# Moving seven output-tile additions in VectorE's order at the start of an MLP

## The reference

```python
def _moe_ref(x, w_in, w_out, a, b):     # x 1152 x 512, w_in 512 x 2048, w_out 2048 x 512
    h = x @ w_in
    h2 = h * h
    h3 = h2 * h
    P = a[0] + a[1] * h + a[2] * h2 + a[3] * h3
    Q = 1.0 + np.abs(b[0]) * np.abs(h) + np.abs(b[1]) * h2
    g = P / (Q + 1e-06)
    return g @ w_out
```

## Time and profile before

| | us |
|---|---|
| median of three runs | 685.32 |
| lowest, highest | 683.48, 688.41 |
| the profiled execution | 685.32 |
| its span (first to last instruction) | 683.5 |
| TensorE busy | 671.2 |
| VectorE busy | 513.4 |
| ScalarE busy | 410.5 |
| GpSimd busy | 443.7 |

### The profile page before, as it was taken

How to read it: one execution, slowest core, us unless ns; L and a number is a source line. 1 busy time by engine, 2 the same in 40 slices (tenths; PEclk the granted TensorE clock), 3 DMA queues, 4 the chain that set the end, 5 groups by cost and what they waited for, 6 DMA issues and landing times.

```text
span 683.5 us, 11834 instructions
## 1 busy us (share of the span) xinstructions
PE 671.2 (98%) x3940; PEld 623.7 (91%) x3940; DVE 513.4 (75%) x1005; ACT 410.5 (60%) x860; POOL 443.7 (65%) x440
## 2 busy tenths in 40 slices
PE   7899999999999999999999999999999999999998
PEld 5899999999999999988999999899999999999996
DVE  6899999999999958989899889977544444444432
ACT  5787887888887878998888888844511111111110
POOL 5877998999999979999789789845614440000000
PEclk9999999999999999999999999999999999999999
DMA  8567467666645430110110110122111100000012
GB/s 230 186 163 205 131 173 220 192 185 156 200 145 159 105 88 3 62 31 32 62 62 0 63 62 5 58 99 87 61 63 62 62 0 1 1 0 1 1 61 78
DMA packets 26012, 60.76 MB, mean 89 GB/s; under 512 B 3304, under 2 KB 7920, under 8 KB 25840
## 3 DMA queue, kind: packets, MB, share of 16 engines
q1 hardware_dynamic: 25680, 59.87, 29.6%
q10 hardware_dynamic: 288, 0.33, 0.2%
HBM read 43.78 MB, written 2.40 MB: 68 GB/s over the span
## 4 chain that ended last, share of the span: by engine, by line
PE 90%; DVE 3%; ACT 2%; DMA 2%; issue 1%; POOL 1%; SPq 0%; DVEq 0%; POOLq 0%; ACTq 0%
PE hb L909 31%; PE ob L966 24%; PE sc L811 11%; PE sc L819 9%; PE misc L837 5%; PE pv_ps L837 5%; PE tb L909 4%; DVE neg_part L1208 1%; DMA km_lo<-kqB 1%; DMA qrawA<-in_q 1%; DVE pt_lo L1217 0%; PE tb L903 0%; ACT num L1104 0%; ACT squares L1132 0%; DMA o_part<-o_sb 0%
## 5 line engine op out<-in xcount | busy, mean ns | idle before, releaser
L1039 ACT ACTIVATE pt_hi<-sc 128x384 fp32r<-128x384 f32 x216 | 90.4, 492 | 46.6 <-PE sc L819 46.6
L1208 DVE TENSOR_REDUCE neg_part<-sc 128x1 f32<-128x384 f32 x216 | 107.7, 549 | 11.5 <-PE sc L811 10.3
L1217 DVE TENSOR_TENSOR pt_lo<-sc,pt_hi 128x384 fp32r<-128x384 f32 x216 | 106.5, 548 | 2.4 <-ACT pt_hi L1039 1.4
L966 PE MATMUL ob<-wo_hi,gt_hi 128*128 128x512 f32 x252 | 99.6, 395 | 0.9 <-issue 0.9
L966 PE MATMUL ob<-wo_lo,gt_hi 128*128 128x512 f32 x252 | 99.2, 394 | 0.0
L966 PE MATMUL ob<-wo_hi,gt_lo 128*128 128x512 f32 x252 | 99.0, 393 | 0.0
L909 PE MATMUL hb<-xt_hi,wi_hi 128*128 128x384 f32 x280 | 94.6, 338 | 0.6 <-DVE xt_lo L1249 0.4
L909 PE MATMUL hb<-xt_lo,wi_hi 128*128 128x384 f32 x280 | 94.1, 336 | 0.0
L909 PE MATMUL hb<-xt_hi,wi_lo 128*128 128x384 f32 x280 | 94.0, 336 | 0.0
L1030 ACT ACTIVATE prob<-sc,neg_max 128x1152 f32<-128x1152 f32 x72 | 89.2, 1238 | 3.2 <-DVE neg_max L1210 3.2
L819 PE MATMUL sc<-ident,prob 128*128 128x128 f32 x648 | 83.1, 273 | 0.6 <-ACT prob L1030 0.6
(11 more groups left out here) (172 smaller groups left out, 1704.0 us busy)
## 6 DMA issues: line engine op xcount, KB each, us to landing
wraw<-in_moe_w_out SPq DMA_DIRECT2D x6, 1024.0 KB, 5.0
krawB<-in_k SPq DMA_DIRECT2D x8, 576.0 KB, 4.4
qrawB<-in_q SPq DMA_DIRECT2D x8, 512.0 KB, 5.7
krawA<-in_k SPq DMA_DIRECT2D x7, 576.0 KB, 4.4
o_part<-o_sb SPq DMA_DIRECT2D x14, 288.0 KB, 4.1
qrawA<-in_q SPq DMA_DIRECT2D x7, 512.0 KB, 5.9
wraw<-in_moe_w_in SPq DMA_DIRECT2D x3, 1024.0 KB, 5.2
wraw<-in_moe_w_gate SPq DMA_DIRECT2D x3, 1024.0 KB, 5.0
```

Source lines behind the costliest of these rows:

```text
L966: ins = nc.tensor.matmul(ob[(m + 1) % 2][:], gt[i][:, f, P * t:P * t + P], wo[c % 2][j][:, f, :], start=f == 0 and n == 0, stop=f == CHUNK ...
L1039: nc.scalar.activation(pt[0][:, 3 * c:3 * c + 3, PT_COL[i]:PT_COL[i] + P], src, ACT.Copy).then_inc(pt_hi, 1)
L1208: nc.vector.tensor_reduce(neg_part[:, s, c:c + 1], sc[s][:, c, 0:KBANK], AX.X, ALU.max, negate=True).then_inc(part_done, 1)
L1217: nc.vector.tensor_tensor(pt[1][:, kt, col], src, pt[0][:, kt, col].bitcast(F32), ALU.subtract).then_inc(pt_lo, 1)
```

## The change

The table of VectorE's turns goes, and `added(u)` is worked out from `behind`: up to u = 8 it takes what stands behind unit u + 1, at u = 9 nothing, and from u = 10 on what stands behind unit u.

```diff
-ADDED_AT = {5: 0, 6: 1, 7: 2, 10: 3, 11: 4, 13: 5, 14: 6}
...
         def added(u):
 
-            if u < 4 * CHUNK:
-                return [(0, ADDED_AT[u])] if u in ADDED_AT else []
-            return behind(u, 0)
+            return behind(u + 1, 0) if u <= 2 * CHUNK else behind(u, 0) if u > 2 * CHUNK + 1 else []
```

## The result

Before 685.18 us (median of 10 runs, 683.48 to 688.41), after 689.20 us (10 runs, 687.85 to 690.89). The ratio is 1.0054, with a 95% interval of 1.0037 to 1.0072: slower by 0.54%, 3.7 us (the medians differ by 4.0). The profiled execution took 688.53 us, 3.2 more than the profiled one of before, with a span of 686.7 against 683.5. The forecast was 687.8, in a range of 684.6 to 690.6.

The account below looks back on a forecast made before the run. TensorE's instruction stream was taken to bound the kernel. Terms +1.64 (tile 2), -0.22 (tile 3's old wait), +2.17 (tile 5) and -1.09 (old wait at 313.26) made +2.5 us on 685.32: 687.8, range 684.6 to 690.6.

Parts of the forecast that it names:

- Two waits: TensorE waits for VectorE's copies about 1.4 us before tile 2 and about 1.9 us before tile 5.
- The old gap at 313 us: TensorE's 0.88 us wait for lo(15) before chunk 1's tile 0 vanishes with its 0.21 restart: -1.09 us.
- GpSimd holds turn 6: activation1(5) waits for GpSimd's second product, so tile 0's copy ends at 276.02 and tile 2 is 1.64 us late.
- ScalarE holds turn 12: activation1(11) follows ScalarE's exponential of unit 11, ended at 294.29, so losing earlier copies makes turn 12 no earlier.
- the first stall: TensorE's stall before tile 2, +1.64 us, drops out of the total because tile 3's copy alone sets tile 5's end.
- the copy of tile 3: At the end of VectorE's turn 12, done at 297.0, it makes tile 5 end 3.59 us late; the largest term.
- The extra copy in turn 8: VectorE's added copy starts turn 9 some 0.6 us later and may push ScalarE by 0.1 to 0.2 us.
- upper bound, 3.7: Likeliest case from above: extra copies of turns 8 and 15 each push the chain by their full 0.6 us.
- The clock: TensorE's clock falls from 2.4 to 1.2 GHz after the stall at 295 us, giving 693 us; chance 0.04.
- near something that cost no clock: Waits of about 1.4 and 1.9 us resemble TensorE's 1.82 us standstill at 18.4 to 20.2 us, clock 1.00.
- Rival 1: VectorE's chain is less tied to ScalarE and GpSimd, both additions arrive in time; 684.0 us at best; chance 0.14.
- Rival 3: Lateness passes from TensorE through ScalarE to VectorE, so tiles 6 to 8 wait some 0.7 us each; 690; chance 0.07.

Follow-up runs that it names:

- the early half alone: Copies of tiles 0 to 2 in turns 6, 7, 8, those of tiles 3 to 6 left as in the kernel before; 684.69 us, ratio 1.0014 to the kernel before.
- the second profile of the changed kernel: Profiled execution of the changed kernel measured again, with nothing altered, beside a variant with added matmuls; median 689.35 us, ratio 1.0053 to the kernel before.
- the late half: Copies of tiles 3 to 6 in turns 12 to 15, those of tiles 0 to 2 left as in the kernel before; 687.94 us, ratio 1.0069.
- the wait of one more turn: Changed kernel with the copies of tiles 3 to 6 one turn later (13 to 16); 695.04 us, ratio 1.0139 to the kernel before.

## Why the prediction was right, and what was missing

**Right.** The direction, the place and the shape. Two waits, both for VectorE's copies: 1.4 us before tile 2 (forecast 1.4) and 2.5 before tile 5 (forecast 1.9). The restart of 0.2 us, seen in the earlier trace rows, is in every one of these products. The old gap at 313 us is gone. GpSimd holds turn 6: activation1(5) began at 273.30, 19.07 us after the mark, against 19.05 before. ScalarE holds turn 12: activation1(11) began at 294.90 after VectorE had idled 0.42 us for the exponential. The statement that the first stall drops out of the total was tested by the early half alone: +0.28 us against +0.3.

**The term that was mis-sized** is the copy of tile 3, "The extra copy in turn 8 may push ScalarE by 0.1 to 0.2; I take 297.0". It was done 43.07 us after the mark, where 297.0 would be 42.43: 0.64 later. Without the turn-8 copy it is 42.15, so that copy and what follows from it cost 0.9, and not 0.1 to 0.2. ScalarE was pushed by 0.88 us, the wait shown above. The step had reckoned with the copy's 0.6 us and the slack: in the same turn VectorE had idled 0.38 us for ScalarE before. It had not asked where the next VectorE instruction with two SBUF inputs would land against GpSimd, which added 0.79 (1.66 against 0.87). By these figures the race is most of the 0.9; this is an estimate, for no run has the copy there without the lost race. The prediction's upper bound, 3.7, was made of full copies and held the +3.07 by luck of size, not by this mechanism.

**The clock** was given 0.04, as a case that had to cost more than 4.4 us to count. That was the wrong way to put it, and the term was put at nothing in the sum. The fall was there in the second profile of the changed kernel and a lower mean clock in 8 of its 12 executions, with some 3.4 us at the lower level and a cost of 1.5 where a profile shows it at tile 5. It belonged into the sum as a term with a chance of its own. The step that both waits "are near something that cost no clock" rested on one execution; in another profile the same wait in the attention, 1.9 us instead of 1.8, was followed by a clock of 0.50. The Trainium skill's rule ("TensorE: Matmul & The Clock Gate", section "The HAM clock gate") that only activity releases the throttle was the better guide. The profiled execution, whose clock stayed at 1.00 (the mean of its span is 1.0), would have confirmed my reading; the second profile of the same kernel shows what the prediction had named as a sign of being wrong, a clock under 1.00 after 295 us. So the median of 689.20 lies in the range, but 1.4 us above the forecast, and most of that is the clock that the sum left out: there the range held by luck.

**Rival 1** (VectorE's chain not tied) is out: the copies came when the chain allowed. **Rival 3** did not happen at this size, but did one turn further on.

The sum as it came out: +2.14 for tile 3's copy in turn 12 (the late half, its clock's 1.55 taken off), +0.92 for the turn-8 copy with the lost race behind it, together the +3.07 of the distance, and nothing for the stall at tile 2. The lower clock comes in 8 executions of 12, which are 2.4 us above the others in the mean, and in the kernel before in 5 of 29, which are 3.6 above the others: 2.4 x 8/12 - 3.6 x 5/29 = 1.0. An execution of the lower kind thus costs more than the 1.5 of one fall; part of that likely lies in a longer wait for the DMA in the attention. With the 2.9 between executions at full clock this makes 3.9, and 3.7 by the ratio and 4.0 by the medians were measured.

## What to carry to other kernels

An in-order engine's place in a written-out order is slack in whole turns: read which addition frees the buffer, in which turn it stands and when that turn can end, and only the latest one counts. A wait on TensorE is to be priced with what follows it: the restart, and by several executions, not one, the clock. And an instruction moved by half a microsecond can change who wins a shared interface, so the next instruction with two SBUF inputs is to be looked up against GpSimd's timeline.

## What the hardware showed

To measure the shared interface by itself, a kernel with VectorE and GpSimd loops only, executed once:

> Only VectorE and GpSimd loops, none of the reference's work. VectorE executes 8 each of: scalar_tensor_tensor of 128 x 384 with both inputs in SBUF and GpSimd idle; the same beside GpSimd products of 128 x 384 back to back; the same with one input in PSUM beside such products; a copy from PSUM beside such products; the first one beside GpSimd memsets. Theory (an instruction of VectorE with two SBUF inputs cannot start reading while a GpSimd instruction that reads SBUF is under way, and ends a fixed 0.41 us after that one's end): 0.61 us alone; up to 1.7 us, and each ending 0.4 us after a GpSimd product's end, in the second group; 0.6 in the third; 0.5 in the fourth; 0.6 in the fifth. Rival (the longer rows are a wait for ScalarE's result that the profile draws into the instruction): 0.61 in all groups of this instruction.

It leaves out all of the reference's work, and took 66.68 us. Groups by line (busy us, mean ns of one, idle before): L143 is the two-SBUF-input instruction alone, L150 beside GpSimd products, L157 with one input in PSUM beside them, L164 a copy from PSUM beside them, L171 the first one beside GpSimd memsets.

```profile
L150 DVE SCALAR_TENSOR_TENSOR res<-h,den 128x384 f32<-128x384 f32 x8 | 9.2, 1146 | 0.3
L171 DVE SCALAR_TENSOR_TENSOR res<-h,den 128x384 f32<-128x384 f32 x8 | 4.5, 559 | 0.2
L143 DVE SCALAR_TENSOR_TENSOR res<-h,den 128x384 f32<-128x384 f32 x8 | 4.5, 558 | 0.3
L164 DVE COPY cop<-bank 128x384 f32<-128x384 f32 x8 | 4.5, 557 | 0.2
L157 DVE SCALAR_TENSOR_TENSOR res<-h,bank 128x384 f32<-128x384 f32 x8 | 4.4, 553 | 0.2
```

Only L150 is longer, 1146 ns in the mean and 1232 in the median, against 553 to 559 in all others. The first of its eight was ahead of GpSimd (553). The numbers expected were somewhat off (0.61 alone, up to 1.7 beside products); the theory's pattern held, and its rival, the same length in all groups, is out. GpSimd pays as well: by its timeline twelve products took 14.32 us beside L150 and 12.79 beside L157. So here a VectorE instruction with two inputs in SBUF ends only after the GpSimd product that was under way when it was issued, and the next product is longer for it; with one input in PSUM, or beside memsets, they don't touch. In the MLP it is the denominator alone that meets this, since VectorE's other operations there read one operand from PSUM.

The second thing is that the fall of TensorE's clock is not read off the length of one wait. The first weight load of tile 5 in the two profiles of the changed kernel, the first and the second, with the idle time ahead of it in brackets:

```profile
297.36 0.19 PEld L963 LDWEIGHTS ob<-wo_hi,gt_hi 128*128 128x128 f32 x1 [2.83 <-DVE tok L1290]
```

```profile
296.97 0.19 PEld L963 LDWEIGHTS ob<-wo_hi,gt_hi 128*128 128x128 f32 x1 [2.82 <-DVE tok L1290]
```

2.83 us kept the clock at 1.00, and 2.82 us led to 0.50, more than a microsecond after work had begun again. The shortest wait in these profiles that was followed by a fall is the 1.9 us in the attention. With the wait of one more turn (6.2 us ahead of the matmul) all five executions have a mean clock of 0.995 or less. Why one execution of the same kernel falls and another does not was not tried.
